# Linear attention on one core: features as the stationary side of key-values, and a column of ones beside the values

## The reference, cut to what matters

```python
def phi(x):                                   # x: batch 4, heads 8, 576 tokens, 64 numbers
    proj = einsum('bhsd,df->bhsf', x, w_phi)  # 128 projections
    proj = proj - max(abs(proj), axis=-1)
    return concatenate([exp(proj), exp(-proj)], -1)   # 256 features
q_p, k_p = phi(q), phi(k)
kv  = einsum('bhsf,bhsd->bhfd', k_p, v)       # 256 x 64 for each head
z   = sum(k_p, axis=2)                        # 256
num = einsum('bhsf,bhfd->bhsd', q_p, kv)
den = einsum('bhsf,bhf->bhs', q_p, z) + 1e-06
x   = num / den                               # rows of 512: 8 heads x 64
x   = moe(x)      # gates x @ w_gate and x @ w_output_gate, the best of 8 experts
out = ffn(x)      # silu(x @ w_in) @ w_out
```

## Time and profile before

| what | value |
|---|---|
| time, median of 3 runs | 886.59 us (884.9 to 886.87) |
| profiled execution, first to last instruction | 885.2 us |
| what lies around that span, against the median | 1.4 us |
| busy: PE, DVE, ACT, POOL | 98%, 63%, 49%, 34% |
| share of the chain that ended last | PE 94%, DVE 2%, the rest 1% or less |
| one turn of attention (one group) | 10.90 us |
| TensorE's granted clock | 0.995 of full over the span |

### The profile page before, as it was taken

The page is one execution under the profiler, slowest core; times in us unless marked ns, Lnnn a source line. Parts: engine busy times, 40 slices in busy tenths (PEclk is TensorE's granted clock), DMA queues, the critical chain, the costliest instruction groups (busy, mean ns, idle before and its releaser), DMA issues.

```text
span 885.2 us, 19077 instructions
## 1 busy us (share of the span) xinstructions
PE 869.3 (98%) x6818; PEld 790.1 (89%) x6819; DVE 559.7 (63%) x837; ACT 433.4 (49%) x793; POOL 298.6 (34%) x264
## 2 busy tenths in 40 slices
PE   7999999989999999999999999999999999999997
PEld 6888888878888888888888899999999999999997
DVE  4777777798704699930370145642568998778882
ACT  5566666553333443434433656655666743333430
POOL 5687776624435545554352210000000011111111
PEclk9999999989999999999999999999999999999999
DMA  5555555416712587551210037645467644444421
GB/s 140 170 157 156 157 155 154 129 29 213 263 49 97 187 259 247 183 156 58 71 47 32 17 94 204 187 117 142 122 196 203 190 145 142 130 133 119 143 73 48
DMA packets 126677, 122.01 MB, mean 138 GB/s; under 512 B 35040, under 2 KB 101728, under 8 KB 126624
## 3 DMA queue, kind: packets, MB, share of 16 engines
q1 hardware_dynamic: 119088, 103.15, 40.0%
q0 software_dynamic: 3504, 11.28, 4.0%
q10 hardware_dynamic: 4032, 6.86, 2.1%
HBM read 86.39 MB, written 34.88 MB: 137 GB/s over the span
## 4 chain that ended last, share of the span: by engine, by line
PE 94%; DVE 2%; SPq 1%; POOL 1%; DMA 1%; issue 0%; ACT 0%; POOLq 0%; DVEq 0%
PE bank L730 24%; PE bank L728 24%; PE bank L729 24%; PE bank L803 4%; PE bank L742 4%; PE bank L756 3%; PE bank L961 3%; PE bank L723 2%; PE bank L783 1%; PE bank L931 1%; PE bank L1000 1%; PE bank L776 1%; PE bank L765 1%; PE bank L905 1%; PE bank L759 1%
## 5 line engine op out<-in xcount | busy, mean ns | idle before, releaser
L711 POOL DMA_INDIRECT out<-temps,ids x18 | 25.1, 1396 | 324.1 <-DVE temps L1650 321.7
L683 POOL TENSOR_TENSOR h_lo<-h_raw,h_hi 128x512 fp32r<-128x512 f32 x49 | 77.8, 1608 | 126.3 <-ACT h_hi L1218 126.3
L728 PE MATMUL bank<-ops,place 128*128 128x384 f32 (+1 forms) x357 | 119.1, 334 | 0.0
L730 PE MATMUL bank<-ops,place 128*128 128x384 f32 (+1 forms) x357 | 118.3, 331 | 0.0
L729 PE MATMUL bank<-ops,place 128*128 128x384 f32 (+1 forms) x357 | 118.3, 331 | 0.0
L1712 DVE TENSOR_TENSOR temps<-temps,bank 128x384 f32<-128x384 f32 x72 | 39.6, 553 | 73.9 <-PE bank L730 73.8
L728 PE MATMUL bank<-place,ops 128*128 128x256 f32 x294 | 83.2, 283 | 0.0
L729 PE MATMUL bank<-place,ops 128*128 128x256 f32 x294 | 83.2, 283 | 0.0
L730 PE MATMUL bank<-place,ops 128*128 128x256 f32 x294 | 83.2, 283 | 0.0
L1621 DVE CAST w_hi<-ahead 128x1024 fp32r<-128x1024 f32 x48 | 52.3, 1089 | 45.1 <-PE bank L730 45.0
L728 PE MATMUL bank<-w_hi,h_hi 128*128 x200 | 80.4, 402 | 0.2 <-issue 0.2
(11 more groups left out here) (251 smaller groups left out, 2168.3 us busy)
## 6 DMA issues: line engine op xcount, KB each, us to landing
ahead<-in_moe_w SPq DMA_DIRECT2D x56, 512.0 KB, 4.5
h_rows<-temps SPq DMA_DIRECT2D x96, 192.0 KB, 2.5
w_raw<-h_rows SPq DMA_DIRECT2D x17, 512.0 KB, 4.1
y_sorted<-y ACTq DMA_DIRECT2D x25, 256.5 KB, 3.2
raw<-h_rows SPq DMA_DIRECT2D x10, 512.0 KB, 3.7
tail<-h_rows SPq DMA_DIRECT2D x9, 512.0 KB, 3.7
qk<-in_k SPq DMA_DIRECT2D x16, 256.0 KB, 3.3
vs<-in_v SPq DMA_DIRECT2D x16, 256.0 KB, 2.9
```

Source lines behind the costliest of these rows:

```text
L683: nc.gpsimd.tensor_tensor(h_lo[:, fs, :], h_raw[:, fs, :], h_hi[:, fs, :].bitcast(F32), ALU.subtract).then_inc(h_lo_done, 1)
L728: mm(o, left_hi, right_hi, start=first, stop=False, skip_group_check=shared)
L730: return mm(o, left_lo, right_hi, start=False, stop=last, skip_group_check=shared)
```

## The change

The two sides of `key_values` are swapped. The features are now stationary, 64 of them at a time, and the values with a 65th column of ones are moving (`DV` = 65), so that kv comes out with features on partitions and z as its last column. For each of 8 slots there are 4 products of 64 x 65, and 4 of 64 x 130 for the mixed slot. VectorE copies this to `kv` (`copy_kv`), now laid out with the two batches' numbers next to each other, so that the numerators read every second word. GpSimd's sums, `key_sums` and the product with the identity go. For the gates alone kv is transposed back (`transpose_kv`, two transposes), copied by ScalarE (`move_kvT`, 256 columns) and multiplied with 32 columns of gate weights (`gates_by_feature`), and ScalarE copies the 64 results in (`move_gates`). `gates_by_feature(g)` stands in the next turn, between `transpose_pairs(n, 0)` and `(n, 1)`. As `vs` has rows of 65 numbers now, v is loaded by two transfers of 512 pieces of 256 bytes instead of one of 256 pieces of 1024 bytes. ScalarE's `move_kvT` moves from between the key features to behind `query_features(g, 1)`; VectorE's `copy_kv` stands ahead of the second `normalize`, where `move_kv` stood behind it.

```diff
+    DV = DH + 1
+    DX = DV + GATES + 1
...
 def load_v(g, par):
...
-                sp.dma_start(vs[par][:, 0:2 * QS, :].rearrange("p (b j) d -> p b (j d)", b=2),
-                             rows[:, 0:QS * P, :].rearrange("b (p j) d -> p b (j d)", j=QS)).then_inc(v_loaded[par], 16)
                 for b in range(2):
-                    sp.dma_start(v_mix[par][64 * b:64 * (b + 1), b, :], rows[b, QS * P:S, :]).then_inc(v_loaded[par], 16)
+                    sp.dma_start(vs[par][:, QS * b:QS * (b + 1), 0:DH],
+                                 rows[b, 0:QS * P, :].rearrange("(p j) d -> p j d", j=QS)).then_inc(v_loaded[par], 16)
+                    sp.dma_start(v_mix[par][64 * b:64 * (b + 1), b, 0:DH], rows[b, QS * P:S, :]).then_inc(v_loaded[par], 16)
...
-            sum_slots(0)
             for g in range(GROUPS):
-                if g < GROUPS - 1:
-                    sum_slots(g + 1)
...
             def key_values(g, par):
                 pe.wait_ge(exp_k_done, 2 * (g + 1))
...
                 for j in range(QS):
                     for b in range(2):
-                        mm(bank[64 * b:64 * (b + 1), ps_kv, 0:2 * F], vs[par][:, QS * b + j, :], phi_k[par][:, QS * b + j, :, :],
-                           start=(j == 0), stop=False)
+                        for c in range(2):
+                            for m in halves:
+                                at = (2 * c + b) * DV
+                                mm(bank[m, ps_kv, at:at + DV], phi_k[par][:, QS * b + j, c, m], vs[par][:, QS * b + j, :],
+                                   start=(j == 0 and b == 0 and c == 0), stop=False, skip_group_check=True)
+                for c in range(2):
+                    for m in halves:
+                        last = mm(bank[m, ps_kv, 2 * c * DV:2 * (c + 1) * DV], phi_k[par][:, K_MIX, c, m],
+                                  v_mix[par][:].rearrange("p b d -> p (b d)"), start=False, stop=True, skip_group_check=True)
+                last.then_inc(kv_done, 1)
+
+            def transpose_kv(g, par):
+                pe.wait_ge(kv_copied, g + 1)
+                for c in range(2):
+                    last = tr(bank[:, ps_kv, KVT + c * F:KVT + (c + 1) * F],
+                              kv[par][:, c, 0:DH, :].rearrange("p d b -> p (d b)"), ident[:])
                 last.then_inc(kvT_done, 1)
-            def key_values_by_feature(g):
+            def gates_by_feature(g):
                 pe.wait_ge(kvT_moved, g + 1)
...
+                    last = mm(bank[:, ps_kv, at:at + 2 * GATES], kvT[:, c, :],
+                              w_head[:, ds(g % H, 1), :, :].rearrange("p a b e -> p (a b e)"), start=True, stop=True)
...
             def numerators(g, par, b, to=ps_num):
-                    pe.wait_ge(kv_moved, g + 1)
+                    pe.wait_ge(kv_ready, 2 * (g + 1))
...
+            def move_gates(g, par):
+                act.wait_ge(gates_done, g + 1)
+                nc.scalar.copy(kv[par][:, :, DV:DV + GATES, :],
+                               bank[:, ps_kv, KVG:KVG + 4 * GATES].rearrange("p (c b e) -> p c e b", c=2, b=2)).then_inc(kv_ready, 1)
...
+            def copy_kv(g, par):
                 dve.wait_ge(kv_done, g + 1)
+                nc.vector.tensor_copy(kv[par][:, :, 0:DV, :],
+                                      bank[:, ps_kv, 0:4 * DV].rearrange("p (c b d) -> p c d b", c=2, b=2)).then_inc(kv_copied, 1)
```

More of the change, by code:

```diff
@@ L115, in build_attention_moe_ffn @@
         qk = [alloc(region, f"qk{i}", [P, 2 * SLOTS, DH]) for i in range(2)]
[L116 to L121, removed]
+        vs = [alloc(region, f"vs{i}", [P, 2 * QS, DV]) for i in range(2)]
+        v_mix = [alloc(region, f"v_mix{i}", [P, 2, DV]) for i in range(2)]
+        kvT = alloc(region, "kvT", [P, 2, F])
+        kv = [alloc(region, f"kv{i}", [P, 2, DX, 2]) for i in range(2)]
         mx = [alloc(region, f"mx{i}", [P, 2, PER_UNIT]) for i in range(2)]
@@ L568, in _ @@
             for i in range(2):
[L569 to L582, removed]
+                step(nc.gpsimd.memset(v_mix[i][:], 0.0))
+                for b in range(2):
+                    step(nc.gpsimd.memset(v_mix[i][64 * b:64 * (b + 1), b, DH:DV], 1.0))
+                step(nc.gpsimd.memset(vs[i][:, :, DH:DV], 1.0))
+            nc.gpsimd.sem_inc(v_ready, 1)
+            nc.gpsimd.memset(w_head[:], 0.0).then_inc(whead_zero, 1)
             nc.gpsimd.memset(lg[:], 0.0).then_inc(lg_zero, 1)
@@ L748, in key_values @@
                 pe.wait_ge(exp_k_done, 2 * (g + 1))
[L749 to L753, removed]
+                pe.wait_ge(v_loaded[par], 4 * 16 * (g // 2 + 1))
+                halves = (slice(0, 64), slice(64, P))
                 for j in range(QS):
                     for b in range(2):
-                        mm(bank[64 * b:64 * (b + 1), ps_kv, 0:2 * F], vs[par][:, QS * b + j, :], phi_k[par][:, QS * b + j, :, :],
-                           start=(j == 0), stop=False)
[L758 to L765, removed]
+                        for c in range(2):
[13 more added lines that the diff above has]
+                              kv[par][:, c, 0:DH, :].rearrange("p d b -> p (d b)"), ident[:])
                 last.then_inc(kvT_done, 1)
-            def key_values_by_feature(g):
+            def gates_by_feature(g):
                 pe.wait_ge(kvT_moved, g + 1)
@@ L825, in attention @@
                 n, npar = g + 1, 1 - par
+                if prev and not nxt:
+                    gates_by_feature(g - 1)
                 if nxt:
@@ L833, in attention @@
                     transpose_pairs(n, npar, 0)
+                    if prev:
+                        gates_by_feature(g - 1)
                     if isinstance(n, int) and n == 0:
                         pe.wait_ge(qk_loaded[0], 5 * 16)
-                    if not (isinstance(g, int) and g <= 0):
-                        pe.wait_ge(kv_moved, g)
                     transpose_pairs(n, npar, 1)
@@ L873, in attention @@
                     transpose_queries(g, par, 1)
[L874 removed]
+                    transpose_kv(g, par)
                     if not nxt:
@@ L878, in attention @@
                         rank_first_half()
+                        gates_by_feature(g)
                 if nxt:
@@ L1152, in attention @@
                     move_pairs(n, 1)
+                if prev:
+                    move_gates(g - 1, npar)
                 if cur and nxt:
@@ L1170, in attention @@
                     query_features(g, par, 1)
+                    move_kvT(g)
                 if cur and not nxt:
                     query_features(g, par, 2)
+                    move_gates(g, par)
             src, at, mix = Q_PART
```

68 lines of the change are left out of this document (20 added, 48 removed).

## The result

The changed kernel takes 895.12 us (median of 4 runs, 892.95 to 897.12), the kernel before 886.73 (4 runs, 884.9 to 887.13): ratio 1.0087, 95% interval 1.0073 to 1.0102. By the ratio it is slower by 7.7 us. The forecast was 886.5, the range ended at 891. The profiled execution has a span of 891.2 us, 6.0 more than before. A turn is named here by the group whose first transposes open it: the turn of group 10 transposes q and k of group 10, makes the key-values of group 9 and the numerators of group 8.

A forecast was written before the change was run, and what follows sets the result against it. Bound: TensorE and a two-turn transfer loop, the loop after the change. Terms -0.7 + 1.7 - 1.0 - 0.1 gave -0.1 us on 885.2, with 1.4 around the span 886.5 us; range 879.5 to 891.

The forecast's parts named there:

- The bound: Attention: the two-turn loop through SyncE's transfers needs 22.14 us, TensorE 20.8; it waits 1.3 us before each even group.
- Key-values: TensorE's key-value products per turn: 2.30 us instead of 2.59, bounds 2.25 and 2.68.
- B: Key-value products: the stationary side costs more, 0.070 us a step, giving 889.8 us; chance 0.17.
- rival C: Key-value products: weight loads do not overlap products, 0.112 us a step, turn of 12.1 us, 905 us; chance 0.02.
- Gates: Two added gate products on TensorE per turn: 0.44 us, 0.49 at the most.
- back to features: TensorE's transposes and products after the numerators: 0.65 us a turn instead of 1.31, saving 0.66.
- E: Gate products wait every turn for a late `move_kvT`; costs little, counted within the forecast's range, no chance of its own.
- SyncE's part: Transfer queue in attention: v's extra issue 0.64 us and +0.15 on the path; a pair of turns grows 0.34.
- the path to the stores: From first transposes to `x_done`: 9.45 us before, +0.15 for added gates less the saving on key-values.
- landing: v's 256-byte pieces land before the weights start: nothing more counted, up to 0.3 us.
- rival D: Numerators reading every second word cost 0.135 us a step instead of 0.070, about +37 us, 923; chance 0.07.
- A: TensorE stays attention's bound, the extra issue hidden: turns equal at 10.4 us, total 879.7 us; chance 0.22.

The follow-up runs named there:

- run 3: Kernel before, with only v's loading changed: two transfers of 256-byte pieces into rows of 65, products as before; 895.06 us, ratio 1.0071.
- run 4: Kernel before, with v in two transfers of whole 1024-byte pieces; 890.04 us, ratio 1.0029.
- run 6: Changed kernel, with GpSimd copying the key-values into a contiguous tile that the numerators read; 897.94 us, ratio 1.0118 to the kernel before.
- run 7: Changed kernel, with q and k issued ahead of the expert weights and v by one transfer, copied by GpSimd; 881.24 us, ratio 0.9931 to the kernel before.
- run 10: Changed kernel, with two tiny transfers that nobody reads issued ahead of each pair of weight chunks; 906.02 us, ratio 1.0205 to the kernel before.
- run 1: Changed kernel, with q and k of even groups issued ahead of the expert weights; 883.12 us, ratio 0.9938 to the kernel before.
- Run 8: Changed kernel, with q and k issued ahead of the weights and numerators reading a contiguous copy by GpSimd; 879.91 us, ratio 0.9922 to the kernel before.

## Why the prediction was wrong

**Right.** The bound (a loop over two turns through SyncE's queue), the place of the wait (before the first transposes of even groups from 4 on, none before odd ones) and what ends it (q). Key-values 2.30 us, predicted 2.30; so 0.058 a step for 64 stationary and 65 moved columns, and rivals B (0.070) and C (no overlap) fall. By the rule of the Trainium skill, TensorE: Matmul & The Clock Gate, "The mechanism", that a weight load overlaps a running product only where the row group differs, the 32 steps of 65 columns would have taken some 3.6 us (rival C's 0.112 each); the trace disagrees with its 118.84 - 116.98 = 1.86. Gates 0.36 (predicted 0.44), back to features 121.72 - 120.99 = 0.73 (0.65). The products of the gates waited for `move_kvT` once, 0.17 us in the last group (E falls). The comparison under GpSimd's subtraction is gone, as predicted.

**The step that failed** is SyncE's part: "v is one issue more: 121.70 - 121.06 = 0.64 us", "I count nothing more, up to 0.3 us", and "+0.15 now" for the path to the stores; together a pair of turns of 22.14. Measured over five pairs: (157.67 - 43.66) / 5 = 22.80, so +1.01 a pair against 21.79 before, instead of +0.34. The missing 0.66, times five 3.3 us, is three terms of one kind, each too small:
- issue: 0.83 instead of 0.64, since the issues behind small pieces get slower too (runs 3 and 4), 0.2;
- landing: q lands 13.02 after the start of the stores instead of 11.90, and of these 1.12 the issues of v are 0.83; the other 0.3 is the term that I had named ("up to 0.3") and valued at nothing. A third of it stands ahead of q's last issue and 0.2 behind it, 3.67 us to the landing instead of 3.47 (0.31 in run 3 against run 4);
- the path to the stores: 9.74 in the mean instead of 9.60, 0.14. This is the stride of the numerators, 0.22 a turn (in run 6, without it, the path is 9.49), less the 0.08 by which the gates are cheaper than the 0.44.

The last is what rival D was about, at a tenth of its price: a stride of two words costs a step 76 ns instead of 70, not 135. The prediction's own sign of D, a run of 81 columns over 1.29 us, did come true with 1.39, and the sum had no term for it. The row that D leaned on the earlier trace rows was misread: its products have 128 stationary columns, and a step of the transposes with as many takes 0.11 too, so that 0.10 needs no stride to explain it. By the Trainium skill, SBUF — State Buffer, "Door 1: The DMA port swizzle", this stride would cost nothing; the trace has 8%.

**What had no step at all** is the clock. I priced a wait at its length. The stretch at 157.6 adds 1.5 us to the turn of group 14, where the sum had -0.5 for each of the last two turns: from there to the last numerators it is 190.35 - 157.67 = 32.68 against 184.21 - 152.60 = 31.61 before, +1.07 instead of -1.0. Of this gap of 2.1 the clock is 1.5, and 0.4 comes from turns that save 0.32 instead of 0.51, by the stride above all. The beginning is the other part: group 2 was to start 1.4 us earlier, it started at 20.94 instead of 21.28, 0.34 earlier, since the record of the granted clock has its higher level from 10.8 us on, before from 5.8 (from 7 to 9.5 us 24 products kept TensorE busy all 2.50 us, where before 25 took 1.68). That is not the change's doing: either kernel shows both. With the changed products group 2 starts at 19.5 to 19.8 where the higher level is there from 5.1 to 6.2 us (runs 6, 7 and 10) and at 20.7 to 21.1 where it comes at 10.5 to 11.1; the kernel before has 22.36 in run 3, with 10.8. Like with like, the 1.4 were about right. Group 4's first transposes came at 43.66, as before (43.67), instead of 0.7 earlier. So the sum stands: 0.0 instead of -0.7, +5.1 instead of +1.7, +1.1 instead of -1.0, and -0.2 at the end: +6.0, the measured difference of the spans.

The median is another 1.7 us above that difference (7.7 to 6.0 by the ratio). The four executions lie at 893.0, 893.3, 897.0 and 897.1, and the profiled one, the first, had a single stretch inside attention. Their mean granted clocks are on record: 0.994, 0.993, 0.990 and 0.989. A stretch of 3.4 us at half clock lowers the mean over this span by 0.2%, so the two long executions have two or three stretches more than the other two, and at 1.5 us each these are about the 4 us. Where in the span they lie isn't shown, since only one execution has a trace.

**Of the rivals**, none came true: the time lies between B (889.8) and C (905). A (TensorE stays the bound, 879.7) is near what happens when q is ahead in the queue: the ratio of run 1 makes 881.2. Run 8 meets A's turn of 10.39 and its time, but it has the stride taken away as well, so that this is partly luck. The range was too narrow above because it took the load loop's error from 5 landings of 0.3 and saw no way in which a longer wait makes the turn itself longer.

## What to carry to other kernels

When an in-order queue has a few tenths of a microsecond of slack per turn, price every issue that the change puts ahead of the late transfer, and take smaller pieces as dearer both in issue and in landing; better, first move what is waited for to the front of the queue, and only then make the engine faster. A wait of TensorE of 1.5 to 3 us may cost more than its length: look in the windows whether the clock falls behind such waits, and count that into the upper bound. A saving on an engine that waits anyway is best tried together with the edit that removes the wait, since alone it can bring nothing or measure as a loss.

## What the runs showed of the hardware

- TensorE's waits of 1.52 to 3.26 us for q were followed by 3.4 us (once 6.8) at the lower clock level in 12 of 23 cases, waits up to 1.48 us in none of 22. Such a stretch costs 1.5 to 1.6 us where TensorE has work throughout.
- A transfer's issue on SyncE takes 0.49 us behind one with 1024-byte pieces and 0.63 behind one with 256-byte pieces, for the same `v_mix` transfer.
- Reading the moving side with a stride of two words: 76 ns a step of 81 columns instead of 70.
- 64 stationary and 65 moved columns in a half of the array: 0.058 us for a pair of instructions; a transpose, with 128 stationary and 128 moved columns, takes 0.11 a step.
- q lands 2.2 to 2.3 us after its last issue where it is ahead of the two 512 KB chunks of weights (run 1, from group 8 on), and 3.4 to 4.1 us behind them (the changed kernel, groups 6 to 14).
